# Other orders of loads, masks and POOL's work in a fused retention and two-layer MLP kernel, and low parts of weights made on VectorE

## What is computed

```python
for t in range(S):
    state = gamma * state + einsum('bhd,bhe->bhde', k[:, :, t], v[:, :, t])
    y[:, :, t] = scale * einsum('bhd,bhde->bhe', q[:, :, t], state)
x = y.transpose(0, 2, 1, 3).reshape(B * S, H * D)

h = x @ w_in;   g = h * cos(h);                 x = g @ w_out      # layer 1
h = x @ w2_in                                                      # layer 2
g = where(h >= 1, h, where(h <= -1, 0, (h + 1)**2 / 4))
out = g @ w2_out
```

## Time and profile before

| | us |
|---|---|
| median of 3 runs | 1112.24 (1111.57 to 1117.05) |
| the profiled execution, its time | 1114.66 |
| its span | 1112.9 |
| PE busy | 1082.4 (97%), 5572 products |
| PE weight loads busy | 888.3 (80%) |
| DVE busy | 682.1 (61%) |
| ACT busy | 515.9 (46%) |
| POOL busy | 232.9 (21%) |
| DMA | 149.12 MB, mean 134 GB/s |

### The profile page before, as it was taken

The page is one execution under the profiler, slowest core; times in us unless marked ns, Lnnn a source line. Parts: engine busy times, 40 slices in busy tenths (PEclk is TensorE's granted clock), DMA queues, the critical chain, the costliest instruction groups (busy, mean ns, idle before and its releaser), DMA issues.

```text
span 1112.9 us, 14425 instructions
## 1 busy us (share of the span) xinstructions
PE 1082.4 (97%) x5572; PEld 888.3 (80%) x5572; DVE 682.1 (61%) x1020; ACT 515.9 (46%) x846; POOL 232.9 (21%) x231
## 2 busy tenths in 40 slices
PE   7899999999999999999999999999999999999998
PEld 5677777877888788788878788888888888888887
DVE  4777774565766546466657577747566656666632
ACT  5577773235666423566654444444332243323332
POOL 4766732330000122000110677600000000000000
PEclk9999999999999999999999999999999999999999
DMA  9445453432333343233224644352233331323111
GB/s 343 137 186 206 170 179 136 152 114 105 133 132 133 104 143 123 105 133 133 86 96 136 243 170 156 137 183 92 104 133 133 133 131 49 121 116 132 67 39 38
DMA packets 44452, 149.12 MB, mean 134 GB/s; under 512 B 4704, under 2 KB 4832, under 8 KB 42336
## 3 DMA queue, kind: packets, MB, share of 16 engines
q1 hardware_dynamic: 44384, 148.20, 37.3%
HBM read 106.24 MB, written 41.94 MB: 133 GB/s over the span
## 4 chain that ended last, share of the span: by engine, by line
PE 74%; ACT 9%; DVE 6%; POOL 4%; DMA 3%; issue 2%; SPq 1%; DVEq 0%; ACTq 0%; POOLq 0%
PE bank L508 10%; PE bank L510 10%; PE bank L512 10%; PE bank L541 8%; PE bank L543 8%; PE bank L542 8%; PE bank L537 6%; PE bank L538 5%; PE bank L539 5%; ACT work L997 2%; ACT work L999 2%; DVE g_lo L753 2%; PE bank L417 2%; DMA kn_sb<-in_k_n 1%; DVE work L723 1%
## 5 line engine op out<-in xcount | busy, mean ns | idle before, releaser
L508 PE MATMUL bank<-x_hi,tw 128*128 128x512 f32 x672 | 264.0, 393 | 8.1 <-DVE late L744 3.9
L510 PE MATMUL bank<-x_lo,tw 128*128 128x512 f32 x672 | 262.2, 390 | 0.0
L512 PE MATMUL bank<-x_hi,tw 128*128 128x512 f32 x672 | 262.0, 390 | 0.0
L537 PE MATMUL bank<-g_hi,wd_hi 128*128 128x512 f32 x384 | 153.4, 400 | 5.4 <-DVE g_lo L753 3.5
L508 PEld LDWEIGHTS bank<-x_hi,tw 128*128 128x128 f32 x672 | 126.5, 188 | 40.0 <-DVE late L744 6.4
L538 PE MATMUL bank<-g_lo,wd_hi 128*128 128x512 f32 x384 | 150.1, 391 | 0.0
L539 PE MATMUL bank<-g_hi,wd_lo 128*128 128x512 f32 x384 | 149.9, 390 | 0.0
L541 PE MATMUL bank<-wd_hi,g_hi 128*128 128x512 f32 x384 | 149.4, 389 | 0.0
L542 PE MATMUL bank<-wd_lo,g_hi 128*128 128x512 f32 x384 | 149.4, 389 | 0.0
L543 PE MATMUL bank<-wd_hi,g_lo 128*128 128x512 f32 x384 | 149.4, 389 | 0.0
L512 PEld LDWEIGHTS bank<-x_hi,tw 128*128 128x128 f32 x672 | 126.5, 188 | 26.6
(11 more groups left out here) (94 smaller groups left out, 1398.8 us busy)
## 6 DMA issues: line engine op xcount, KB each, us to landing
tw<-t_scratch SPq DMA_DIRECT2D x64, 896.0 KB, 6.4
t_scratch<-tw SPq DMA_DIRECT2D x16, 1792.0 KB, 7.4
work<-x_scratch SPq DMA_DIRECT2D x24, 256.0 KB, 3.5
raw<-in_w1u SPq DMA_DIRECT2D x16, 256.0 KB, 3.2
wd_raw<-in_w1d SPq DMA_DIRECT2D x8, 512.0 KB, 8.8
q_sb<-in_q_t SPq DMA_DIRECT2D x16, 256.0 KB, 2.9
k_sb<-in_k_t SPq DMA_DIRECT2D x16, 256.0 KB, 3.8
v_sb<-in_v_n SPq DMA_DIRECT2D x16, 256.0 KB, 4.1
```

Of the source, the lines that this page charges most:

```text
L508: nc.tensor.matmul(to[:, :], w[:, kt, 0, i, :], x_hi[:, i, kt, :], start=opens, stop=False, skip_group_check=True)
L510: nc.tensor.matmul(to[:, :], w[:, kt, 0, i, :], x_lo[:, i, kt, :], start=False, stop=False, skip_group_check=True)
L512: last = nc.tensor.matmul(to[:, :], w[:, kt, 1, i, :], x_hi[:, i, kt, :], start=False, stop=kt == 1, skip_group_check=True)
L537: nc.tensor.matmul(to[i][:, :], wd_hi[:, f, cols], g_hi[:, slot, :], start=opens, stop=False)
```

## The change

1. **Loads at the start.** SP loads for unit u its q and k, then v and k_n of unit u - 1. The first weights come behind k of the last unit. `load_columns` is split in `load_q` and `load_k`; the k of a later unit waits for the scores two units back instead of the outputs.
2. **Start on the engines.** DVE scales q of unit 2 too. Masks 6 and 7 stand inside `operands`, behind the x sum and ahead of the low part. POOL makes x3's operand before the low parts of the second weights; the last state update stands in quad 0.
3. **Quads.** In quads 1 to 6 of spans 0 and 3 DVE makes the low parts of the next quad's weights, one behind `sum_h22` and one behind gate 1; `gate_low` stands behind `angle` 1. ACT makes `wd_high` of the next quad behind `curve` 1. In quad 1 `copy_p1` is first and waits for u2.
4. **POOL's operations.** A low part of 896 elements is split in 512 and 384, one of down weights in two of 512.
5. **Tails.** One gate_low goes ahead of `angle` 2, one ahead of gate 3, with their high parts on ACT, and one ahead of the last x sums.
6. **Layer 2's first weights.** Those of its quads 0 and 1, and down weights 0, are made in the tail of span 2 (`MADE_LATE`), and quad 1's are loaded there.

Here is SP at the program's start, before; `late` and `first_in` hold the units' tiles. First units 0 to 2, from the first load behind those of q and k of unit 1.

The diff, cut to its core:

```diff
+MADE_LATE = [2, 3, 9, 10]
@@ SP
-                if not first and u % AHEAD >= 2:
-                    sp.wait_ge(y_done, u - 1)
-                sp.dma_start(unit_k(u), columns(k_t[u]))
+            def load_k(u):
+                if not first and u % AHEAD >= 2:
+                    sp.wait_ge(scores_done, 2 * (u - 1))
+                sp.dma_start(unit_k(u), columns(k_t[u]))
...
+            for u in range(2, AHEAD):
+                load_q(u)
+                load_k(u)
+                load_v(u - 1)
+                load_kn(u - 1)
+            load_weights(0)
...
-                    if n < QUADS * SPANS:
+                    if n < QUADS * SPANS and not (q == 0 and s >= PAIRS):
                         load_weights(n)
...
                 elif s + 1 < SPANS:
                     load_x2(s + 1, 0)
+                    load_weights(QUADS * (s + 1) + 1)
...
                     for i in range(2, AHEAD):
-                        load_columns(u + i)
+                        load_k(u + i)
+                        load_q(u + i)
+                        load_kn(u + i - 1)
                         load_v(u + i)
-                        load_kn(u + i)
@@ DVE
                     x_sum(s, "s3", kt)
+                    if s == 0:
+                        mask(i + 2)
                     split_low(s, "p7", kt)
...
+                    if lows:
+                        gate_low(s - 1, *lows.pop(0))
                     x_sum(s, "s2", kt)
...
-                angle(s, q, 2)
                 if q == QUADS - 1:
                     gate_low(s, *TAIL[1])
+                angle(s, q, 2)
...
+                if s == 0 and q == 0:
+                    update_state(AHEAD - 1)
+                more = made(s) and 0 < q < QUADS - 1
                 sum_h22(s, q)
+                if more:
+                    t_low(weight_item(QUADS * s + q + 1, 0))
                 if q == 0:
                     gate(s, q, 0)
+                angle(s, q, 1)
                 gate_low(s, 1, q)
-                angle(s, q, 1)
                 gate(s, q, 1)
+                if more:
+                    t_low(weight_item(QUADS * s + q + 1, 1))
...
                 gate(s, QUADS - 1, 2)
+                gate_low(s, *TAIL[2])
                 gate(s, QUADS - 1, 3)
-                gate_low(s, *TAIL[2])
@@ ACT
+                elif q == 1:
+                    act.wait_ge(u2_done, n)
...
+                if q == 1:
+                    copy_p1(s, q)
                 if q:
                     finish_turns(s, q - 1)
...
-                more = 1 < n < QUADS * SPANS and made(n // QUADS)
+                more = made(s) and 0 < q < QUADS - 1
...
-                if made(s):
-                    wd_high(s // PAIRS, q)
                 curve(s, q, 1)
+                if made(s) and q + 1 < QUADS:
+                    wd_high(s // PAIRS, q + 1)
...
+                        if s == PAIRS - 1:
+                            if n in MADE_LATE:
+                                t_high(weight_item(QUADS * PAIRS, 0) + MADE_LATE.index(n))
+                            if n == len(tail) - 1:
+                                wd_high(1, 0)
@@ POOL
+                for part in (slice(0, 4), slice(4, 7)):
+                    last = nc.gpsimd.tensor_tensor(tw[half][:, kt, 1, part, :], ...)
...
+                if s == PAIRS - 1:
+                    for n in (QUADS * PAIRS, QUADS * PAIRS + 1):
+                        t_sums(weight_item(n, 0))
+                        t_sums(weight_item(n, 1))
+                        t_low(weight_item(n, 0))
+                        t_low(weight_item(n, 1))
+                    wd_low(1, 0)
```

131 lines of the change are left out of this document (66 added, 65 removed).

## The result

The changed kernel takes 1106.29 us (median of six runs, 1105.6 to 1107.2), the kernel before 1112.78 in runs beside it: a ratio of 0.9931, 95% interval 0.9909 to 0.9953. It is faster, by 6.5 us, where 15 were forecast, and it lies above the range. The two profiled executions are 1114.66 and 1106.12 us with spans of 1112.9 and 1104.3, so there are 8.6 us to account for between these two; the profiled execution of before is 1.9 us over its median, so the medians are nearer to each other.

A forecast was written before the change was run, and what follows sets the result against it. The prediction took TensorE (PE) as the bound, so only its gaps could be won. Terms 3.8 + 2.7 + 4.3 + 0.9 + 4.1 - 0.7 = 15.1 us gave a median of 1097.1 us, range 1092.0 to 1105.5.

The forecast's parts named there:

- The load of k between spans: Between spans 0 and 1: k of unit 10 no longer waits, and the clock recovers, together 2.7 us sooner.
- The waits for layer 2's first weights: PE's two waits at 626 and 628 us go and the clock there recovers: 4.1 us sooner.
- One DVE low part of 896 elements: Quads of span 0: each new DVE low part takes 1.0 us by elements, rows expected at 1.1, bounds 0.69 to 2.17.
- Rivals 1 and 2: Span 0's quads: shorter loop, PE alone sets them, 1093.7 us (0.12); POOL's wd_low ahead of DVE's second low part, 1103.4 (0.12).
- I charge 0.7 (0 to 3): Tail of span 2: new POOL sums and low parts beside DVE's SBUF instructions cost 0.7 us, bounds 0 to 3.
- The rival on collisions: Third rival, tail of span 2: POOL's sums hold DVE 0.46 us each, costing 3 us instead of 0.7; 1099.4 us, chance 0.10.
- I get the first product at 38.3: Start: the first product of quad 0 comes at 38.3 us instead of 40.19, 1.9 us sooner.
- the gain at the first down product is 2.4: Quad 0 of span 0: POOL ends x3's low parts about 4 us sooner, the first down product comes 2.4 us sooner.
- rival 4: Start gives nothing: ACT's wait for k_n idles PE over 3 us, the clock falls, 2.4 us lost; 1099.5 us, chance 0.06.
- the term of span 0: Start, quad 0 and quads of span 0: span 0 ends 1.8 + 1.4 + 0.6 = 3.8 us sooner.
- g_lo and copy_p1: Five g_lo waits in tails of spans 0 to 2: 4.3 us sooner; copy_p1 made before the turns in quad 1: 0.9.
- The forecast of 15.42 us: DVE and ACT loop per quad of span 0, from 15.70 us: -1.48 without POOL's hold, -0.60 by order, +2.0 for new low parts.

The follow-up runs named there:

- k_alone: The kernel before with only the loads between spans changed: k with its own wait, k_n behind q; 1113.31 us in one run, against 1114.78 for the kernel before.
- t_high_2_sooner: The changed kernel, but ACT makes the third high part of the first weights during the start, behind the operands of unit 6; 1107.6 us in one run.
- x3_dve: The changed kernel, but DVE instead of POOL makes x3's operand and its low parts in span 0; 1104.51 us in one run.
- kn_behind: The changed kernel, but ACT scales k_n of each unit one place later, so output copies don't stand behind a load; 1103.61 us in one run.
- four: The changed kernel with the edits of pool_quads, dve_tail, kn_behind and x3_dve together; 1095.82 us, ratio 0.9838 to the kernel before.
- pool_quads: The changed kernel, but POOL makes the weights' low parts in quads 1 to 6 as before, in halves, the new order kept; 1101.59 us.
- dve_tail: The changed kernel, but DVE makes the low parts of layer 2's first weights in span 2's tail, POOL keeps the sums; 1102.12 us.
- tail_as_before: The changed kernel, but layer 2's weights of quads 0 and 1 are made where they were before, down weights 0 stay in the tail; 1106.32 us.

## Why the prediction was off

**Right.** The load of k between spans (2.7 forecast, 2.66 measured; no wait for `k_sb` near 194, clock at 1.00). The waits for layer 2's first weights (4.1, 4.2). One DVE low part of 896 elements (1.1 forecast, 1.08) and with it one quad per 15.43 us, 15.42 forecast, waiting at the second half of p1 as said (0.19 at 87.58). Rivals 1 and 2 did not come. A gap does cost more than its idle time, by 0.27 us, where I took 0.25: 0.98 idle at 586.38 is 1.14 over the pace, and the next product comes 0.11 late as well; in span 0 a gap of 0.19 idle makes a quad of 14.96 one of 15.43. Of the 4.2 us at layer 2's first weights 0.8 was luck of the pair: in k_alone, whose code there is that of before, the clock doesn't fall behind the waits, and the stretch is 0.8 us shorter.

**Wrong, the largest: the step "I charge 0.7 (0 to 3)" for the tail of span 2.** It measured 4.4, above its own upper bound of 3. The rival on collisions counted sums against DVE at 0.46 each and compared the backlog with 1.4 us of slack. It left out POOL's low parts, 128x512 and over a us each, which the sum had named for the same place, and that the price isn't paid once. Four of them in a row beside four DVE instructions took 6.10 us: DVE gets one instruction of 0.69 us through per 1.5 us, while the tail asks for up to four per 2.7. The slack is used up within one down group. The page "SBUF — State Buffer" of the Trainium skill, section "Who interferes with whom", was weighed for this very place and its rule of a lock for a whole instruction is what the rows show (1.50, 1.78, 0.94 for 0.69). The rule was right; the price that I put on it was too low. The row that I had should have led there: in the earlier trace rows one DVE instruction took 2.17 beside one of POOL, and four of POOL's in a row are four such holds. The third rival named this mechanism, and its 3 us were nearer; but it went by the sums alone, and only two of the four gaps, 1.2 of the 4.4 us, stand where POOL is at the sums.

**Wrong: the steps "I get the first product at 38.3" and "the gain at the first down product is 2.4".** The first held where the clock did (38.2 to 38.6 in three profiles of that start code) and not in the profile of the changed kernel (39.37). There ACT's wait for k_n, seen in the text and given a rival of its own (rival 4, 0.06), left PE idle for 2.37 us, and the clock stood at 0.66 behind it. That wait is in the traces of all the kernels with this order, but the clock fell behind it only in some, so the rival came in a mild form and in part. The second step failed outright: 0.1 instead of 2.4. It took x3's low parts to end about 4 us sooner; they ended 1.5 us sooner (48.35 instead of 49.84), and quad 0 took 16.96 us up to its first down product where the forecast left it 15.7. In the trace after, POOL's x3 operands lie beside DVE's low parts of x and both stretch, ACT's turns stand behind POOL's x3 and the high parts of weights, and the first `gate_low` lies beside `wd_low`. From there the missing 2 us went through to the loops: they begin 0.2 us later, where the forecast had 1.8 sooner, and that is what the term of span 0 lacks. How the 3 us of waiting in quad 0 divide between DVE held by POOL and ACT's order stays open: t_high_2_sooner mended one and worsened the other, and in x3_dve and kn_behind longer waits and a lower clock came in instead. In four the first down product comes at 54.75, the earliest seen.

**Wrong in the small: g_lo and copy_p1.** At 243 us the new place of `gate_low` ends one wait, and the next item waits 0.49 us at 245.36 in its stead. `copy_p1` first removes the wait of p7 but the down product behind it now waits 0.42 us for its own `g_lo` (267.83 and 462.63): 0.7 instead of 0.9. In both, "what comes next" was priced too low: 0.9 us in all.

**Right in size and wrong in worth: the loop.** The forecast of 15.42 us took DVE's new low parts as given and did the sum around them. Its own terms named what pool_quads measured: -1.48 and -0.60 from POOL's absence and from the order, +2.0 from the new work. That most of the -1.48 was to be had without the +2.0, with POOL meeting `gate_low` for 0.45 us only, wasn't asked. And the wait that DVE's low part brings in quad 2 (2.01 us at 72.14) was no part of it: in dve_tail, tail_as_before and t_high_2_sooner the clock fell behind it (0.70 to 0.81 granted in 70 to 75 us), which cost 1.1 to 1.6 us more.

## What to carry to other kernels

Work that is moved "where POOL is idle" isn't free where DVE is busy on the path. Look first at which of DVE's instructions there read both inputs from SBUF. Count each of these that meets POOL as POOL's own time and half a us, and compare the sum with what the stretch asks of DVE, not one instruction with its slack. Here the same work cost DVE half of POOL's time. It was better on DVE in a stretch with room (the tail), and better on POOL in one whose length is a loop through DVE (the quads), where it met the loop's instructions only at an edge. And time won ahead of a stage is worth what the stage's first wait leaves of it: look at what stands last there before adding it up.

## What the runs showed of the hardware

A DVE instruction with both inputs in SBUF and a POOL instruction that reads SBUF take turns, one by one, as long as both engines have such work. A DVE row of 0.69 us becomes 0.94 beside a POOL 128x128 of 0.46, 1.50 beside a 128x384 of 1.02, 1.78 beside a 128x512 of 1.27 and 2.58 to 2.61 beside a 128x896 of 2.14: POOL's own time and 0.4 to 0.5. POOL's halves take 1.46 and 1.75 in place of 1.02 and 1.27. A DVE instruction with an input in PSUM isn't touched: in the thirteen traces over 1800 rows of 128x512 with such an input run beside POOL's, and none takes more than 0.75 us.

Cutting POOL's instruction in two shortens the longest hold (waits of 0.98 and 1.48 us instead of 1.70 and 2.30) and leaves the time that DVE loses as it is (3.8 us over two low parts, either way).

A wait of PE among products of 128x512, at the full clock, costs 0.27 us more than its idle time: 0.16 at the product that waited and 0.11 at the next.

The same code's start differs by up to 2.6 us between executions (first product at 38.2 to 40.2 us for the changed kernel's, 40.19 and 42.82 for that of before), with a granted clock of 0.50 to 1.00 in the stretch that varies. That is as much as several of the edits here are worth, and behind waits of about 2 us later on the clock fell in some executions and not in others. Edits there are judged by more than one profile, or by the time between the same two products further on: the tail of span 2 took 34.27 to 34.32 us in five profiles.
